# First head pair loaded raw, stacked and split on chip; first layer job spread over more slots

## The reference

```python
# q, k, v: (4 batches, 8 heads, 576 tokens, 64), fp32
scores = (1 / 8) * q @ k.T
kth = the 32nd largest of each row
attn = softmax(where(scores >= kth, scores, -1e9))
x = (attn @ v), laid out as 2304 tokens x 512
g = curve(x @ moe_w_in)            # 0 below -1, h above 1, (h + 1)**2 / 4 between
x = g @ moe_w_out                  # w_in 512 x 2048, w_out 2048 x 512
out = relu(x @ moe2_w_in) ** 2 @ moe2_w_out
```

## Time and profile before

| what | value |
|---|---|
| median of 3 runs | 1306.61 us (1305.96 to 1307.04) |
| the profiled execution, its own time | 1310.51 us |
| its span in the trace | 1308.7 us |
| mean granted TensorE clock | 0.957 of full |
| PE busy | 1204.5 us, 92% |
| PE weight loads | 1141.5 us, 87% |
| DVE busy | 907.9 us, 69% |
| POOL busy | 781.6 us, 60% |
| ACT busy | 718.4 us, 55% |

### The profile page before, as it was taken

How to read it: one execution, slowest core, us unless ns; L and a number is a source line. 1 busy time by engine, 2 the same in 40 slices (tenths; PEclk the granted TensorE clock), 3 DMA queues, 4 the chain that set the end, 5 groups by cost and what they waited for, 6 DMA issues and landing times.

```text
span 1308.7 us, 24410 instructions
## 1 busy us (share of the span) xinstructions
PE 1204.5 (92%) x8760; PEld 1141.5 (87%) x8760; DVE 907.9 (69%) x2014; ACT 718.4 (55%) x1591; POOL 781.6 (60%) x636
## 2 busy tenths in 40 slices
PE   1477799899899999999999999999999999999998
PEld 1466798799789999999999999999989999999887
DVE  3799889989889998988889999989861111111111
ACT  1455576576465566677666664546542565642332
POOL 0799778787787867686767667666662222222222
PEclk9955799799899999999999999999999999999999
DMA  6698865865777992452436852345419500680000
GB/s 204 225 349 293 276 227 193 284 226 191 276 253 289 366 367 65 163 167 83 149 107 237 312 215 64 116 149 201 158 60 351 225 33 1 258 322 3 31 17 17
DMA packets 98872, 246.15 MB, mean 188 GB/s; under 512 B 7360, under 2 KB 48320, under 8 KB 86464
## 3 DMA queue, kind: packets, MB, share of 16 engines
q1 hardware_dynamic: 98752, 244.59, 53.0%
HBM read 167.49 MB, written 77.07 MB: 187 GB/s over the span
## 4 chain that ended last, share of the span: by engine, by line
PE 70%; POOL 9%; ACT 7%; DVE 7%; issue 3%; DMA 3%; SPq 1%; ACTq 0%; POOLq 0%
PE h_ps L535 27%; PE y_ps L556 14%; PE y_ps L550 12%; PE pv_ps L497 6%; PE tr_ps L470 4%; POOL s_sb L963 3%; DVE top L800 3%; PE score_ps L435 3%; POOL prob L968 2%; DVE rest L802 2%; DMA kq_lo<-in_kq_dram 1%; POOL w_out L955 1%; ACT prob L641 1%; PE pv_ps L509 1%; PE pv_ps L492 1%
## 5 line engine op out<-in xcount | busy, mean ns | idle before, releaser
L535 PE MATMUL h_ps<-xt_hi,w_in 128*128 128x256 f32 x2304 | 480.0, 291 | 9.4 <-ACT r_sb L705 3.4
L981 POOL TENSOR_TENSOR g_lo<-g_sb,g_hi 128x256 fp32r<-128x256 f32 x288 | 219.2, 761 | 413.5 <-ACT g_hi L719 413.3
L535 PEld LDWEIGHTS h_ps<-xt_hi,w_in 128*128 128x128 f32 x2304 | 381.7, 193 | 16.1 <-ACT r_sb L707 4.7
L535 PE MATMUL h_ps<-xt_lo,w_in 128*128 128x256 f32 x1152 | 327.6, 284 | 0.0
L800 DVE MAX8 top<-rest 128x8 f32<-128x576 f32 x432 | 303.9, 744 | 0.0
L963 POOL TENSOR_SCALAR s_sb<-s_sb,top 128x576 f32<-128x576 f32 x144 | 257.5, 1788 | 55.2 <-DVE top L800 54.2
L550 PE MATMUL y_ps<-g_hi,w_out 128*128 128x256 f32 x1152 | 231.7, 284 | 1.0 <-POOL g_lo L981 0.8
L719 ACT ACTIVATE g_hi<-g_sb 128x256 fp32r<-128x256 f32 x288 | 120.8, 420 | 195.4 <-DVE g_sb L854 77.4
L535 PEld LDWEIGHTS h_ps<-xt_lo,w_in 128*128 128x128 f32 x1152 | 222.5, 193 | 2.3
L802 DVE MATCH_REPLACE8 rest<-top,rest 128x576 f32<-128x576 f32 x288 | 211.5, 741 | 0.0
L556 PE MATMUL y_ps<-w_out,g_hi 128*128 128x512 f32 x576 | 204.0, 396 | 0.1
(11 more groups left out here) (69 smaller groups left out, 1691.8 us busy)
## 6 DMA issues: line engine op xcount, KB each, us to landing
w_in<-w_scratch SPq DMA_DIRECT2D x32, 1024.0 KB, 6.8
w_out<-w_scratch SPq DMA_DIRECT2D x32, 1024.0 KB, 8.2
ks<-ks_scratch SPq DMA_DIRECT2D x48, 576.0 KB, 5.5
qs<-qs_scratch SPq DMA_DIRECT2D x80, 256.0 KB, 4.8
stage<-in_w_dram SPq DMA_DIRECT2D x32, 512.0 KB, 4.7
w_scratch<-w_in SPq DMA_DIRECT2D x16, 1024.0 KB, 8.8
w_scratch<-w_out SPq DMA_DIRECT2D x16, 1024.0 KB, 7.6
v_sb<-in_vv_dram SPq DMA_DIRECT2D x48, 325.0 KB, 5.9
```

What stands on the lines that cost most here:

```text
L535: last = pe.matmul(h_ps[:, 0:CHUNK], wi[:, f // 2, w, m, cols], x[:, m, :], start=(m == 0 and n == 0), stop=(m == KT - 1 and n == 2))
L981: pool.tensor_tensor(g_lo[k % 2][:, :], g_sb[k % 2][:, :], g_hi[k % 2][:, :].bitcast(F32), ALU.subtract).then_inc(g_lo_done, 1)
```

## The change

- The k and q of the first pair that slots 0 and 1 need come a second time in the input, as `kq0`: each head's 64 rows once in partitions 0 to 63 and once in 64 to 127, 576 columns of k and 256 of q for each head. Two DMAs put them raw into `prob[0]` and `prob[1]`, which are free until the first exponential. ScalarE writes `hi` straight into `ks[0]`, `qs[0]` and `qs[1]` (one copy of 128 x 576 and four of 64 x 128 for each head), VectorE subtracts `lo` (one of 64 x 576 and four of 64 x 128 for each head). Slots 0 and 1 wait for that instead of for the DMAs from DRAM.
- The order of the preps becomes pair 1, 2, 3, 0, 4, ...: pair 0 is still needed from slot 8 on. One prep instead of two stands ahead of slot 0. `PREP_SLOT` becomes (-1, 0, 2, 4, 7, 9, 13, 15, 17, 28, 30, ...), the first layer's weights take the slots 0 to 12 as (1, 2, 1, 2, 1, 2, 1, 1, 1, 1, 1, 1, 1).
- Job 0 takes two positions in three from position 33 on: 31, 33, 34, 36, 37, ..., 52, 54. Its result is copied at position 56. `SOON` is empty and `turned_before` equals `x_slot`, so these do nothing.

```diff
+PREP_ORDER = (1, 2, 3, 0, 4, 5, 6, 7, 8, 9, 10, 11, 12, 13, 14, 15)
-PREP_SLOT = (-2, -1, 0, 2, 5, 8, 10, 14, 16, 18, 30, 32, 38, 41, 44, 47)
+PREP_SLOT = (-1, 0, 2, 4, 7, 9, 13, 15, 17, 28, 30, 32, 38, 41, 44, 47)
-W1_PER_SLOT = (1, 1, 1, 2, 1, 1, 1, 2, 1, 1, 1, 1, 1, 1)
+W1_PER_SLOT = (1, 2, 1, 2, 1, 2, 1, 1, 1, 1, 1, 1, 1)
...
+    for _f in range(FT):
+        UP_POS.append(_q)
+        _q += 1
+        if _j == 0 and _q >= 30 and _q % 3 == 2:
+            _q += 1
+START = UP_POS[::FT]
+FINAL = [q + 2 for q in UP_POS[FT - 1::FT]]
...
+            def load_first():
+                for t in range(2):
+                    sp.dma_start(prob[t][:, 0:F_HEAD],
+                                 kq0[:, F_HEAD * t:F_HEAD * (t + 1)]).then_inc(first_loaded[t], 16)
...
+            load_first()
             load_kq(0)
+            load_v(0, 0, 0)
             stage_block(0)
             restack(0)
-            load_slot_ks(0)
-            load_slot_qs(0)
-            load_slot_qs(1)
             load_kq(1)
-            restack(1)
-            load_kq(2)
...
+                    if n < 2:
+                        pe.wait_ge(first_lo, (5 * t + 3, FIRST_LO)[n])
...
+            def split_first(t):
+
+                act.wait_ge(first_loaded[t], 16)
+                act.activation(ks[0][:, t, :], first_k(t), ACT.Copy).then_inc(first_hi, 1)
+                for a in range(2):
+                    for var in range(2):
+                        rows = slice(DIM * var, DIM * (var + 1))
+                        act.activation(qs[a][rows, t, var, :], first_q(t, a)[rows, :],
+                                       ACT.Copy).then_inc(first_hi, 1)
...
+                    if n < 2:
+                        act.wait_ge(first_lo, FIRST_LO)
...
+            split_first(0)
+            split_first(1)
+            copy_scores(0, 0)
+            copy_scores(0, 1)
             split_kq(0)
-            copy_scores(0, 0)
-            split_kq(1)
-            copy_scores(0, 1)
...
+            def split_first(t):
+
+                dve.wait_ge(first_hi, 5 * t + 1)
+                low = slice(DIM, P)
+                dve.tensor_tensor(ks[0][low, t, :], first_k(t)[low, :], ks[0][low, t, :].bitcast(F32),
+                                  ALU.subtract).then_inc(first_lo, 1)
+                for a in range(2):
+                    dve.wait_ge(first_hi, 5 * t + 3 + 2 * a)
+                    for var in range(2):
+                        rows = slice(DIM * var, DIM * (var + 1))
+                        dve.tensor_tensor(qs[a][rows, t, 1 - var, :], first_q(t, a)[rows, :],
+                                          qs[a][rows, t, var, :].bitcast(F32),
+                                          ALU.subtract).then_inc(first_lo, 1)
...
+            split_first(0)
+            split_first(1)
             split_kq(0)
-            split_kq(1)
...
+    for hh in range(2):
+        both = kq[0, 0, hh::2, 0:F_HEAD]
+        kq0[:, F_HEAD * hh:F_HEAD * (hh + 1)] = np.concatenate([both, both])
```

More of the change, by code:

```diff
@@ L25 @@
 VW = 5 * 2 * V1
+F_HEAD = SEQ + 2 * P
+FIRST_LO = 10
 SLOTS = 72
@@ L45 @@
 DIRECT = 2
-START = []
+SOON = []
+UP_POS = []
 for _j in range(len(JOBS)):
-    START.append(FIRST[_j] if _j in FIRST else START[-1] + FT)
+    _q = FIRST.get(_j, UP_POS[-1] + 1 if UP_POS else 0)
+    for _f in range(FT):
[5 more added lines that the diff above has]
+FINAL = [q + 2 for q in UP_POS[FT - 1::FT]]
 SETS = []
@@ L54 @@
 SET_OF = {_j: s for s, js in enumerate(SETS) for _j in js}
-UP_AT = {START[j] + f: FT * j + f for j in range(len(JOBS)) for f in range(FT)}
+UP_AT = {q: k for k, q in enumerate(UP_POS)}
 DOWN_AT = {q + 2: k for q, k in UP_AT.items()}
 READ_AT = {START[j] - 1: j for j in range(DIRECT, len(JOBS))}
-COPY_AT = {START[j] + FT + 1: j for j in range(len(JOBS))}
+COPY_AT = {q: j for j, q in enumerate(FINAL)}
 JOB_OF = {lc: j for j, lc in enumerate(JOBS)}
@@ L115, in by_vector, with turned_before @@
     return i >= WBLOCKS and i % 2 == 1
+def turned_before(c):
+    return x_slot(c)
 def packed(n):
@@ L133, in batch_pair, with build @@
     return c // 2, (n % 8) // 2
-def build(nc, kq, vv, w_raw, out):
+def build(nc, kq, kq0, vv, w_raw, out):
     def scratch(name, shape):
@@ L200, in build @@
         w_staged = [sem(f"w_staged{i}") for i in range(2)]
+        first_loaded = [sem(f"first_loaded{i}") for i in range(2)]
+        first_hi = sem("first_hi")
+        first_lo = sem("first_lo")
         w_hi_done = sem("w_hi_done")
@@ L257, in wait_block_ready, with first_k, first_q @@
                 eng.wait_ge(w_moved[i], 16 * (s + 1))
+        def first_k(t):
+            return prob[t][:, 0:SEQ]
+        def first_q(t, a):
+            return prob[t][:, SEQ + P * a:SEQ + P * (a + 1)]
         block = ctx.enter_context(nc.Block())
@@ L263, in _, with load_kq, restack @@
         def _(sp):
-            def load_kq(g):
-                if g:
-                    sp.wait_ge(restacked, 16 * 6 * g)
+            def load_first():
+                for t in range(2):
+                    sp.dma_start(prob[t][:, 0:F_HEAD],
+                                 kq0[:, F_HEAD * t:F_HEAD * (t + 1)]).then_inc(first_loaded[t], 16)
+            def load_kq(at):
+                g = PREP_ORDER[at]
+                if at:
+                    sp.wait_ge(restacked, 16 * 6 * at)
                 sp.dma_start(kq_lo[:, :].bitcast(F32), kq[g // PAIRS, g % PAIRS]).then_inc(kq_loaded, 16)
-            def restack(g):
-                sp.wait_ge(kq_hi_done, g + 1)
-                sp.wait_ge(kq_lo_done, g + 1)
+            def restack(at):
+                g = PREP_ORDER[at]
+                sp.wait_ge(kq_hi_done, at + 1)
+                sp.wait_ge(kq_lo_done, at + 1)
                 for x, part in enumerate((kq_hi, kq_lo)):
@@ L376, in slot @@
                         load_slot_ks(n // 2 + 1)
-                    load_slot_v(n // 2)
+                    if n:
+                        load_slot_v(n // 2)
                 if n + 2 < NORMAL:
@@ L427, in score @@
                 if not packed(n):
[L428 to L431, removed]
+                    if n < 2:
+                        pe.wait_ge(first_lo, (5 * t + 3, FIRST_LO)[n])
+                    elif n % 2 == 0:
+                        pe.wait_ge(ks_loaded[(n // 2) % 2], 16 * (n // 4 + (n // 2) % 2))
+                    if t == 0 and n >= 2:
+                        pe.wait_ge(qs_loaded[n % 2], 16 * (n // 2))
                     kk, qq = ks[(n // 2) % 2], qs[n % 2]
@@ L902, in slot @@
             def slot(n):
-                here, past = n < SLOTS, 0 <= n - 2 < SLOTS
+                here, past = n < SLOTS, 0 <= n - 2 < SLOTS and n - 2 not in SOON
                 def both(op):
@@ L933, in slot @@
                 at(3 * n + 2)
+                if n - 1 in SOON:
+                    add_to_total(n - 1)
+                    invert_total(n - 1)
+                    scale_pv(n - 1)
+            split_first(0)
+            split_first(1)
             split_kq(0)
-            split_kq(1)
             for n in range(SLOTS + 2):
@@ L1016, in lay_out @@
     kq = np.zeros((b, PAIRS, P, KQ), np.float32)
+    kq0 = np.zeros((P, 2 * F_HEAD), np.float32)
     vv = np.zeros((b, PAIRS, P, VW), np.float32)
@@ L1049, in lay_out @@
             blocks.append(x.transpose(1, 0, 2).reshape(P, 1024))
-    return kq, vv, np.ascontiguousarray(np.stack(blocks))
+    return kq, kq0, vv, np.ascontiguousarray(np.stack(blocks))
 def kernel(**inputs):
@@ L1063 @@
     arrays, args = {}, []
-    for name, a in (("kq", kq), ("vv", vv), ("w", w)):
+    for name, a in (("kq", kq), ("kq0", kq0), ("vv", vv), ("w", w)):
         arrays[f"in_{name}_dram"] = a
```

20 lines of the change are left out of this document (10 added, 10 removed).

## The result

The changed kernel takes 1294.48 us (median of 4 runs, 1293.39 to 1295.3) against 1306.82 (median of 4, 1305.96 to 1307.69): a ratio of 0.9898, 95% interval 0.9879 to 0.9916. Forecast was 1293.7, in a range of 1286 to 1303. Its profiled execution took 1293.4, with a span of 1291.6.

What follows compares the result with a forecast made beforehand. GpSimd's list and a two-slot loop were taken to set the pace before about 257 us, TensorE (97% busy) after it. Terms 12.5 - 4.0 + 9.4 - 5.0 = 12.9 us off 1306.6 gave 1293.7, range 1286 to 1303.

Steps and rivals of the forecast that it cites:

- Part 1: Start, up to the first mask of slot 0: without the six DMAs ahead of the first scores, a gain of 12.5 us.
- M(0): M(n) is the first instruction of mask(n, 0) on GpSimd; for slot 0 forecast at 30.6 us, before 43.1.
- Part 2: Slots 1 to 9: GpSimd's longer list of blocks and preps costs 4.0 us, bounds 0 and 7.
- M(9): GpSimd's first mask instruction of slot 9; forecast near 131 us, before 139.7.
- The two waits of the loop: Slots 6 and 8, one block alone: the loop over two slots through the other engines binds, costing 1.2 to 1.5 each.
- the wait for kq_hi in slot 2: GpSimd's wait in slot 2, 1.2 us before, shrinks to 0.9.
- rival D: Late DMAs eat the start: slots 1 to 9 cost 10, the later part 7; sum 5, 1302 us; chance 0.11.
- Part 3: Slots 10 to 18: prep gone from slot 10, two-step slots at 11.4 us; sum 107.8, a gain of 9.4.
- M(18): GpSimd's first mask instruction of slot 18; forecast near 239 us, before 257.0.
- rival C: Slots 11 to 17: two-step slots come only from 13.5 to 12.5 us; sum 5.2, 1301 us; chance 0.12.
- Part 4: From slot 18 on: job 0's late copy, store and stage, and slot 28's prep, lose 5 us, bounds 0 and 10.
- Rival B: Slots 11 to 17: clock does not hold with two steps a slot; 18.9 us a slot, 1346 worst case; chance 0.09.

Runs made afterwards that it cites:

- prep_in_10: The changed kernel with the prep of slot 9 put back into slot 10; 1296.35 us, ratio 0.992 to the kernel before.
- weight_first: The changed kernel with slot 0's weight block ahead of its prep on ScalarE and GpSimd; 1291.35 us, ratio 0.988.
- prep_first: The changed kernel with kq_hi of the first prep ahead of the score copies on ScalarE; 1291.65 us, ratio 0.9879.
- glo_split: The changed kernel with GpSimd's preps and weight blocks ahead of the slot's last g_lo and their instructions cut in two; 1296.9 us, ratio 0.9924.
- both_first: The changed kernel with kq_hi of the first prep ahead of the score copies and slot 0's weight block ahead of its prep; 1288.29 us, ratio 0.9859.
- ends_54: The changed kernel with job 0 at three steps a slot from position 48 on, its result copied at 54; 1295.45 us, ratio 0.9905.
- three_steps: The changed kernel with job 0 back at three steps a slot, positions 31 to 46, copied at 48; 1294.91 us, ratio 0.9905.
- steps_alone: The kernel before with nothing changed but job 0's new positions; 1307.95 us against 1307.13, ratio 0.9997.

## Why the prediction was right, and where it was not

**Part 1, the start: right.** 12.5 forecast, 12.1 at the first MAX8 and 12.0 at M(0). Two errors nearly cancelled: the first raw load landed by 4.0, 0.6 earlier than drawn, and the small copies took 0.32 each (four in 1.29) against 0.25 drawn. The first scores so came on time (6.26), but the copies of the second head kept ScalarE until 7.8, 0.2 too late for the first score copy; that is more than half of the 0.35 by which the first MAX8 is late.

**Part 2, slots 1 to 9: right mechanism, a little too dear.** M(0) to M(9) took 99.3, forecast 100.7, before 96.7: a loss of 2.6, not 4.0. The two waits of the loop in slots 6 and 8 came as said (1.5 and 1.3); the wait for kq_hi in slot 2, for which 0.9 was charged, vanished, and that is most of the 1.4 too much. ScalarE's kq_hi in slot 4 did not wait for its load, so rival D did not appear; in `prep_in_10`, `weight_first` and `prep_first` it waited 0.6, 0.5 and 0.3 us, so the margin is as thin as forecast.

**Part 3, slots 10 to 18: half of it failed.** The forecast was 107.8 for M(9) to M(18), the trace has 111.0: a gain of 6.2 instead of 9.4. Its first term, the prep that leaves slot 10, held (4.3 against 3.9, and 4.1 when it was put back). Its second did not: seven slots at 11.4 us were forecast from the one old slot with two steps and nothing new in it, and they took 86.5 instead of 79.8. Only the slots without a prep or block keep that pace (11.2); with one they take 12.4 to 13.0, so the mean is 12.4. That is rival C, with the reason given there, and its objection, that a block just fits, was wrong: a block or prep lengthens the slot although GpSimd has that much idle time in it. That this is for the moment at which GpSimd gets to it, behind the last g_lo, is not shown: put ahead of that g_lo and cut in two (`glo_split`), it still made slots of 12.8, though there it held VectorE for 0.8 us. I had also taken the old M(10) to M(17), 86.4, for slow; it already held two easy slots (16 and 17, without steps), so evening out gained nothing there. M(17) to M(18) gave the rest: 11.3, where 14.4 had been feared and 13.4 measured before; the clock in that slot was 1.00, and 0.86 before, a term that the forecast did not have.

**Part 4, later: did not happen.** Loss of 5 forecast. M(18) to M(71) took 707.9 us before and 707.8 after. M(18) to M(19) is 0.8 longer and slot 28, with its prep, 1.6; slots 20 to 27 gave that back. The stage of slot 19 landed 0.9 us before ScalarE needed it.

So the total (12.9 forecast; 12.3 by the medians, 13.3 by the ratio) is right partly by luck: part 3 was 3.2 too high and part 4 5 too low. At M(18) the traces say 15.5, forecast 17.9; at M(71) they say 15.6, forecast 12.9. That this is more than the medians give is in part the high execution in which the kernel before was profiled.

**The clock.** Slots 12 to 17 ran at 1.00 throughout, with PE busy 63.4 of 74 us. Slot 11 did not (0.90 in 143 to 156): the step whose matmuls start at 142.4 runs at half speed until 145.3 (0.41 us for a single one, 0.28 after that), 2 us behind a stretch in which TensorE stood still for 2.3 us, from 137.9 to 140.3. Rival B appeared for these 3 us alone, and slot 11 took 12.8 us, where `both_first` and `ends_54` have 12.4 at 1.00. The Trainium skill's rule ("TensorE: Matmul & The Clock Gate", "What's actually happening") that a clock is throttled by default and released by activity did not bite in slots 12 to 17. Thinning the steps even kept the clock in slots 16 to 18, where it fell without it (`three_steps`).

**Left open.** Which wait sets the 13.0 us of a slot with a prep: with GpSimd's work moved it was 14.1 (VectorE's new wait) and 12.8 with that cut in two, with ScalarE's moved 13.0 to 13.3. And why the kernel before's profiled execution was 3.9 above its median: 1.5 of it lie behind M(71), the rest has no place yet; the trace of `steps_alone`, nearly the same kernel, has a span of 1306.3. The new start was never run without the moved preps, so that its 12 us reach the end is shown by the milestones and by the two moves ahead of slot 1, not by taking it away.

## What to carry to other kernels

When a list of one engine (here GpSimd's masks, preps and blocks) and a loop through the others bind at nearly the same pace, write both down per slot; that gave the milestones within a microsecond up to M(9), and M(10) within 1.4. Before a pace is taken from one slot, list what else that slot had to do: the "two steps" slot was fast because it had no prep. The prep ahead of the first step of the pipeline cost 4.1 us there, of which 3.3 were left at M(71); shortening the chain of the start was passed on to the end in full, and each link of it (what stands ahead of kq_hi, what stands between the load and the mask) is worth a look.

## What the runs showed of the hardware

VectorE's instruction with two SBUF inputs (128 x 256, 0.41 us) took 2.25 to 2.51 us when it met GpSimd's long instruction with two SBUF inputs, and 0.96 to 1.20 when that was cut in two. The Trainium skill says this ("SBUF — State Buffer", "Who interferes with whom"): a VectorE instruction with two SBUF inputs contends with a GpSimd instruction that reads SBUF, and the port pair that they share is an exclusive lock. The traces agree: VectorE's ended 0.3 us behind GpSimd's. The lock was at work without these moves too: in the changed kernel the same instruction takes 1.22 us at 184.05, where GpSimd multiplies the mask until 185.0, and in the kernel before 1.76 at 170.23. I had looked at GpSimd's idle time as free; here it was free only where VectorE had no such instruction.

The granted clock of the changed kernel's trace is 0.99 in 31 to 130 us, where the kernel before shows 0.64 (43 to 140) and 0.50 (98 to 131); yet the matmuls there are as slow as in the kernel before (four of the scores 1.31 us, in the first row, as at 98.7 in the kernel before, against 0.70 in the second, at full clock), so the record of the clock misses this stretch. The mean clock of such a trace (0.994 here, 0.957 before) therefore says nothing on which kernel had the faster TensorE. Timeline of PE, changed kernel:

```profile
35.17 1.31 PE L469 MATMUL score_ps<-ks,qs 128*128 128x288 f32 x4
...
195.51 0.70 PE L469 MATMUL score_ps<-ks,qs 128*128 128x288 f32 x4
```
